# An xLSTM cell in chunks: scores and carried state by two heads at a time on halves of TensorE's rows, q loaded once, narrow matmuls streamed up to 128 columns wide

## The reference, cut to what matters

```python
B, H, S, D = 4, 8, 768, 40
for t in range(S):
    m_new = maximum(f_gate[:, :, t] + m, i_gate[:, :, t])
    f_stab = exp(f_gate[:, :, t] + m - m_new)
    i_stab = exp(i_gate[:, :, t] - m_new)
    m = m_new
    C = f_stab * C + i_stab * outer(v[:, :, t], k[:, :, t])   # 40 x 40 per head
    n = f_stab * n + i_stab * k[:, :, t]
    h = C @ q[:, :, t]
    y[:, :, t] = sigmoid(o_gate[:, :, t]) * h / maximum(abs(n @ q[:, :, t]), 1.0)
x = y as (B * S, H * D)         # 3072 x 320
logits = x @ w_gate             # then routing, experts, second network
```

## Time and profile before

| | |
|---|---|
| median of 3 runs | 818.24 us (818.19 to 818.46) |
| the profiled execution | 816.46 us |
| its span, first to last instruction | 814.7 us |
| PE / PEld busy over the span | 766.5 us (94%) / 719.1 us (88%) |
| DVE / ACT / POOL busy | 585.3 us (72%) / 323.2 us (40%) / 170.4 us (21%) |
| this stage (24 tiles) | about the first 180 us |

### The profile page before, as it was taken

How to read it: one execution, slowest core, us unless ns; L and a number is a source line. 1 busy time by engine, 2 the same in 40 slices (tenths; PEclk the granted TensorE clock), 3 DMA queues, 4 the chain that set the end, 5 groups by cost and what they waited for, 6 DMA issues and landing times.

```text
span 814.7 us, 17195 instructions
## 1 busy us (share of the span) xinstructions
PE 766.5 (94%) x5535; PEld 719.1 (88%) x5535; DVE 585.3 (72%) x1614; ACT 323.2 (40%) x775; POOL 170.4 (21%) x244
## 2 busy tenths in 40 slices
PE   5999999985389999999999999999999999999995
PEld 4999999973378998999899889989998998999995
DVE  5767677776767876887788678768867876884442
ACT  4656566520223442361345145323613442362331
POOL 8257677510100110021002102100210110021001
PEclk9999999965599999999999999999999999999998
DMA  6887887510500500230041005004100500230000
GB/s 157 221 227 214 234 214 215 139 40 2 171 1 1 162 27 10 77 95 24 0 142 29 24 14 157 24 0 141 29 24 0 161 26 8 80 91 25 2 1 24
DMA packets 73408, 65.79 MB, mean 81 GB/s; under 512 B 35232, under 2 KB 64544, under 8 KB 73376
## 3 DMA queue, kind: packets, MB, share of 16 engines
q1 hardware_dynamic: 63584, 51.94, 23.0%
q0 software_dynamic: 2688, 8.65, 3.4%
q10 hardware_dynamic: 7104, 4.79, 1.9%
HBM read 56.71 MB, written 8.65 MB: 80 GB/s over the span
## 4 chain that ended last, share of the span: by engine, by line
PE 91%; DVE 5%; DMA 1%; issue 1%; POOL 0%; ACT 0%; ACTq 0%; DVEq 0%; POOLq 0%
PE bank L835 20%; PE bank L837 18%; PE bank L836 18%; PE bank L677 6%; PE bank L724 5%; PE bank L853 4%; PE bank L854 4%; PE bank L705 2%; PE bank L712 2%; PE bank L688 2%; PE bank L878 1%; PE bank L879 1%; PE bank L669 1%; PE bank L758 1%; PE bank L733 1%
## 5 line engine op out<-in xcount | busy, mean ns | idle before, releaser
L835 PE MATMUL bank<-wo_hi,h_hi 128*128 128x320 f32 x384 | 120.8, 314 | 0.0
L837 PE MATMUL bank<-wo_hi,h_lo 128*128 128x320 f32 x384 | 118.6, 309 | 0.0
L836 PE MATMUL bank<-wo_lo,h_hi 128*128 128x320 f32 x384 | 118.0, 307 | 0.0
L601 POOL DMA_INDIRECT xe<-x_rows,idx_in x24 | 30.5, 1272 | 403.2 <-DVE idx_in L1434 353.9
L1494 DVE SCALAR_TENSOR_TENSOR g_act<-g_neg,rest_alpha,bank 128x384 f32<-128x384 f32 x128 | 78.6, 614 | 39.2 <-ACT g_neg L1066 37.7
L1066 ACT ACTIVATE g_neg<-bank 128x384 f32<-128x384 f32 x128 | 62.8, 491 | 102.0 <-PE bank L854 102.0
L1070 ACT CAST h_hi<-g_act 128x384 fp32r<-128x384 f32 x128 | 65.7, 513 | 78.8 <-DVE g_act L1494 78.3
L1064 ACT ACTIVATE h_hi<-bank 128x384 fp32r<-128x384 f32 x64 | 31.5, 492 | 163.4 <-PE bank L854 163.4
L835 PE MATMUL bank<-yT_hi,wi_hi 128*128 128x384 f32 x256 | 92.3, 361 | 0.3 <-DVE yT_lo L1520 0.3
L836 PE MATMUL bank<-yT_lo,wi_hi 128*128 128x384 f32 x256 | 86.8, 339 | 0.0
L837 PE MATMUL bank<-yT_hi,wi_lo 128*128 128x384 f32 x256 | 86.7, 339 | 0.0
(11 more groups left out here) (229 smaller groups left out, 1816.1 us busy)
## 6 DMA issues: line engine op xcount, KB each, us to landing
s<-w SPq DMA_DIRECT2D x8, 1280.0 KB, 9.2
s<-w SPq DMA_DIRECT2D x8, 1024.0 KB, 5.5
s<-w SPq DMA_DIRECT2D x16, 256.0 KB, 6.3
k_in<-kT SPq DMA_DIRECT2D x24, 160.0 KB
q_wide<-qT SPq DMA_DIRECT2D x48, 80.0 KB
k_row<-k SPq DMA_DIRECT2D x24, 160.0 KB, 3.4
v_in<-v SPq DMA_DIRECT2D x24, 160.0 KB, 4.0
gate_o<-o SPq DMA_DIRECT2D x24, 160.0 KB, 3.1
```

The lines of the kernel that those rows point to most:

```text
L835: pe.matmul(acc, ah, bh, start=start, stop=False, skip_group_check=True)
L836: pe.matmul(acc, ah, bl, start=False, stop=False, skip_group_check=True)
L837: return pe.matmul(acc, al, bh, start=False, stop=stop, skip_group_check=True)
```

## The change

Rows 0 to 63 of TensorE hold the even head of a pair, rows 64 to 127 the odd one (`half_rows`, `head`). The scores are 8 matmuls on 64 rows each, alternating between the halves, 128 columns into a bank for each half. The carried part is 8 matmuls on 64 rows, alternating, each streaming 123 columns (its own 41 and the next 82, which later matmuls overwrite), one half into CARRY and the other into the UPD bank, behind the state's update. The update is 8 matmuls with 40 columns loaded and 41 streamed, on all rows, whose results land on partitions 0 to 39 or 64 to 103. Because the carried part now writes the bank UPD, the wait for `state_ready` moves ahead of it. q is loaded once, into `q_in`; `q_wide`, `own_half` and their memsets go. The outputs stream 128 columns instead of 41, the logits 96 (12 copies) instead of 8. VectorE reads the carried part in two operations, and writes the state in one of 164 columns on 128 partitions.

```diff
@@ sp
-                sp.dma_start(k_in[0:PD, b, :, :], kT[c, b].rearrange("u d y s -> (u d) y s")).then_inc(qk_in[b], 16)
-                for half in range(2):
-                    sp.dma_start(q_wide[D * half:D * half + D, b, half, :, :], qT[c, b, half]).then_inc(qk_in[b], 16)
...
+                for u in range(2):
+                    sp.dma_start(k_in[ROWS * u:ROWS * u + D, b, :, :], kT[c, b, u]).then_inc(qk_in[b], 16)
+                for u in range(2):
+                    sp.dma_start(q_in[ROWS * u:ROWS * u + D, b, :, :], qT[c, b, u]).then_inc(qk_in[b], 16)
...
                 if not first(T, B):
-                    for half in range(2):
-                        sp.dma_start(q_in[D * half:D * half + D, b, :, :].rearrange("d (a u) s -> d a u s", u=2),
-                                     qT[c, b].rearrange("u d (a n) s -> n d a u s", n=2)[half]).then_inc(q_rows_in[b], 16)
@@ pool, constants
             pool.memset(k_in[:, 1, :, :], 0.0)
-            pool.memset(q_wide[:, 1, :, :, :], 0.0).then_inc(wide_zero, 1)
-            pool.memset(k_row[:, :, DM:], 0.0)
-            pool.memset(v_in[:, :, :, D:D1], 1.0).then_inc(consts, 1)
+            pool.memset(q_in[:, 1, :, :], 0.0).then_inc(wide_zero, 1)
+            pool.memset(v_in[:, :, H:, :], 0.0)
+            pool.memset(state[:, :, :], 0.0)
+            pool.memset(v_in[:, :, 0:H, D:D1], 1.0).then_inc(consts, 1)
...
-            pool.memset(q_in[:, :, :, :], 0.0)
-            pool.memset(state[:, :, :, :], 0.0)
...
@@ pool, weigh_values
-                pool.tensor_tensor(fstate[:, n, :, :], state[0:PD, b, :, :], bc(fade[:, c, b, :], 2 * D1),
+                pool.tensor_tensor(fstate[:, n, :, :], of_batch(b), bc(fade[:, c, b, :], D1),
                                    ALU.mult).then_inc(faded, 1)
@@ pe, front
                 for y in range(HP):
-                    ins = pe.matmul(SCORE[y // 2][:, 2 * P * (y % 2):2 * P * (y % 2) + 2 * P], k_in[:, b, y, :],
-                                    q_wide[:, b, :, y, :], start=True, stop=True)
+                    for u in range(2):
+                        ins = pe.matmul(SCORE[u][:, P * y:P * y + P], k_in[half_rows(u), b, y, :], q_in[half_rows(u), b, y, :],
+                                        start=True, stop=True)
@@ pe, router
-                    ins = pe.matmul(YB[:, H * D1:H * D1 + E], xT_sb[:, t, :], wg_sb[:, t, :],
-                                    start=(t == 0), stop=(t == 2))
+                    ins = pe.matmul(LOGITS.rearrange("p (n e) -> p n e", e=E), xT_sb[:, t, :],
+                                    wg_sb[:, t, :].unsqueeze(1).to_broadcast([P, LOGIT_COPIES, E]), start=(t == 0), stop=(t == 2))
@@ pe, back
+                if not first(T, 1) and (not isinstance(T, int) or T <= NT - B):
+                    pe.wait_ge(state_ready, T)
...
                 for y in range(HP if not first(T, B) else 0):
-                    pe.matmul(pair(CARRY[:, 0:H * D1].rearrange("p (h d) -> p h d", d=D1), y), q_in[:, b, y, :], state[:, b, y, :], start=True, stop=True)
+                    for u in range(2):
+                        pe.matmul(CARRIED[u][:, D1 * y:D1 * y + 3 * D1], q_in[half_rows(u), b, y, :],
+                                  state[half_rows(u), HP * b + y:HP * b + y + 3, :].rearrange("p y d -> p (y d)"), start=True, stop=True)
                 pe.wait_ge(kv_in[b], 32 * (c + 1))
                 if not final(T):
                     pe.wait_ge(vw_ready, T + 1)
-                    if not first(T, 1):
-                        pe.wait_ge(state_ready, T)
                 for y in range(HP if not final(T) else 0):
-                    pe.matmul(UPD[:, 2 * D1 * y:2 * D1 * (y + 1)], k_row[:, b, 2 * D * (y // 2 + 2 * (y % 2)):2 * D * (y // 2 + 2 * (y % 2)) + P],
-                              pair(vw[:, n, :, :], y), start=True, stop=True)
+                    for u in range(2):
+                        pe.matmul(UPDATE[ROWS * u:ROWS * u + D, D1 * y:D1 * y + D1], k_row[:, b, D * (HP * u + y):D * (HP * u + y) + D],
+                                  vw[:, n, head(u, y), :], start=True, stop=True)
...
-                        ins = pe.matmul(YB[:, D1 * h:D1 * h + D1], probs[:, n, half, y, :], v_in[:, b, h, :], start=True, stop=True)
+                        h, at = head(half, y), D1 * (HP * half + y)
+                        ins = pe.matmul(YB[:, at:at + WIDE], probs[:, n, half, y, :],
+                                        v_in[:, b, :, :].rearrange("p h d -> p (h d)")[:, D1 * h:D1 * h + WIDE], start=True, stop=True)
@@ dve, make_x
-                    ch.link(dve.tensor_tensor(carried[:, :, :], grid(CARRY), bc(gT[:, c, hs], D1), ALU.mult))
+                    for u in range(2):
+                        ins = dve.tensor_tensor(of_half(carried[:, :, :], u), CARRIED[u][:, 0:HP * D1].rearrange("p (y d) -> p y d", d=D1),
+                                                of_half(bc(gT[:, c, hs], D1), u), ALU.mult)
+                        ch.mark(ins) if u == 0 else ch.link(ins)
...
-                            ins = dve.scalar_tensor_tensor(out=state[0:PD, b, :, cols], in0=new, scalar=own_half[:, half:half + 1],
-                                                           in1=fstate[:, n, :, cols], op0=ALU.mult, op1=ALU.add)
+                        ins = dve.tensor_tensor(of_batch(b), new, fstate[:, n, :, :], ALU.add)
```

More of the change, by code:

```diff
@@ L48, in build_program @@
     REST = DM - 2 * P
-    PD = 2 * D
+    ROWS = P // 2
     J1, J2 = F1 // P, F2 // P
@@ L191, in build_program @@
         wT = ga("wT", [P, NCH, HB])
-        fade = ga("fade", [PD, NCH, B, HP])
-        state = ga("state", [P, B, HP, 2 * D1])
+        fade = ga("fade", [P, NCH, B, HP])
+        state = ga("state", [P, B * HP + 3, D1])
         q_in = ga("q_in", [P, B, HP, P])
-        q_wide = ga("q_wide", [P, B, 2, HP, P])
         k_in = ga("k_in", [P, B, HP, P])
-        k_row = ga("k_row", [P, B, DM + P - PD])
+        k_row = ga("k_row", [P, B, DM])
         gate_o = ga("gate_o", [P, B, DM])
-        own_half = ga("own_half", [PD, 2])
-        v_in = ga("v_in", [P, B, H, D1])
+        v_in = ga("v_in", [P, B, H + 3, D1])
         vw = ga("vw", [P, 2, H, D1])
@@ L360, in pieces_before, with half_rows, head, of_half @@
             return sum(len(first_pieces(i)) for i in range(n))
+        def half_rows(u):
+            return slice(ROWS * u, ROWS * u + ROWS)
+        def head(u, y):
+            return 2 * y + u
+        def of_half(heads, u):
+            return heads.rearrange("p (y u) d -> p u y d", u=2)[:, u, :, :]
+        def of_batch(b):
+            return state[:, HP * b:HP * b + HP, :]
         def bc(ap, n):
@@ L486, in _ @@
             pool.memset(k_in[:, 1, :, :], 0.0)
-            pool.memset(q_wide[:, 1, :, :, :], 0.0).then_inc(wide_zero, 1)
-            pool.memset(k_row[:, :, DM:], 0.0)
-            pool.memset(v_in[:, :, :, D:D1], 1.0).then_inc(consts, 1)
+            pool.memset(q_in[:, 1, :, :], 0.0).then_inc(wide_zero, 1)
+            pool.memset(v_in[:, :, H:, :], 0.0)
+            pool.memset(state[:, :, :], 0.0)
+            pool.memset(v_in[:, :, 0:H, D:D1], 1.0).then_inc(consts, 1)
             for b in range(2, B):
                 pool.memset(k_in[:, b, :, :], 0.0)
-                pool.memset(q_wide[:, b, :, :, :], 0.0).then_inc(wide_zero, 1)
-            pool.memset(q_in[:, :, :, :], 0.0)
-            pool.memset(state[:, :, :, :], 0.0)
[L495 to L502, removed]
+                pool.memset(q_in[:, b, :, :], 0.0).then_inc(wide_zero, 1)
+            ch.link(pool.memset(half_ones[:, :, :], 0.0))
+            pool.memset(half_ones[:, 0, half_rows(0)], 1.0)
+            pool.memset(half_ones[:, 1, half_rows(1)], 1.0).then_inc(consts, 1)
             ch.link(pool.memset(ones_bf[:, :], 1.0))
@@ L667, in front @@
                     for y in range(HP):
-                        h = H * b + HP * half + y
+                        h = H * b + head(half, y)
                         ins = pe.matmul(LOGD[half][:, P * y:P * y + P], sel3[:, h:h + 1].to_broadcast([P, P]),
@@ L1106, in _ @@
             dve.memset(k_in[:, 0, :, :], 0.0)
-            dve.memset(q_wide[:, 0, :, :, :], 0.0).then_inc(wide_zero0, 1)
+            dve.memset(q_in[:, 0, :, :], 0.0).then_inc(wide_zero0, 1)
+            ones_done.mark(dve.memset(UPDATE, 0.0))
             ones_done.mark(dve.memset(peak3[3 * HB:P, :], 0.0))
@@ L1251, in read_logits @@
                 dve.wait_ge(logit_done, T + 1)
-                dve.tensor_copy(logits[:, T, :], YB[:, H * D1:H * D1 + E]).then_inc(logit_read, 1)
+                dve.tensor_copy(logits[:, T, :], LOGITS[:, 0:E]).then_inc(logit_read, 1)
             def make_x(c, b):
@@ L1256, in make_x @@
                 n = b % 2
-                ch = Chain(dve, dve_step, STEP_LINKS * T - (T if first(T, B) else B))
+                ch = Chain(dve, dve_step, STEP_LINKS * T - 2 * (T if first(T, B) else B))
                 hs = slice(H * b, H * b + H)
```

(20 more changed lines are left out.)

41 lines of the change are left out of this document (20 added, 21 removed).

## The result

The median of four runs of the changed kernel is 797.54 us (796.16 to 799.48), beside 818.35 us for the kernel before on the same chip: a ratio of 0.9742, 95% interval 0.9717 to 0.9768. The profiled execution took 797.02 us, where the prediction's sum gave 797.4.

The account below looks back on a forecast made before the run. TensorE was taken to set the loop's pace. Start -6.0, T = 4 to 19 -12.0 (15 rounds of 6.05 us) and end -1.1 took 816.46 us to 797.4, or 799 as median of runs; range 790 to 832.

Parts of the forecast that it names:

- Two halves at once: Scores and carried part on TensorE: halves overlap at 56 ns a matmul, -0.89 us for scores, +0.05 for carried part.
- rival 1: Halves don't overlap; scores and carried matmuls pay 112 ns each, round 7.74 us, total 832 us; chance 0.24.
- Three switches at 0.12 us: Changes between full and half height in TensorE's round: three, together +0.36 us, range 0.2 to 0.45.
- Update 0.58: State's update on TensorE: 16 instructions loading 40 columns take 0.58 us instead of 0.89, -0.31 a round.
- Widening 0: Wider outputs, logits and carried part stay under the load's time: 0 a round, with 0.1 us kept in the range.
- TensorE's round 5.96: Sum of TensorE's terms for one round in the loop: 5.96 us, from 6.75.
- The moved wait just fits: Carried part now waits for the state: ready at about 112.24 us, TensorE there at 112.28.
- Rival 3: VectorE, ScalarE and GpSimd bound the round above 6.05 us; at 6.5 us a round, 806 us; chance 0.10.
- Start -2.6 and -3.4 of clock: Until T = 4: fewer memsets and shorter first scores give -2.6 us, full clock -3.4; together -6.0.
- q once 0: Loading q once saves 160 KB and two issues a tile, off the path: 0.
- Rival 2: Half an overlap, 84 ns each: 6.75 + 0.05 in the loop, only start and clock gains remain, 814 us; chance 0.12.
- Rival 4: TensorE's clock falls more often with 64 rows working; each 3.4 us at half costs 1.7, eleven eat the gain; chance 0.04.

Follow-up runs that it names:

- same_half_in_a_row: The changed kernel with scores and carried part issuing all matmuls of one row half before the other, instead of alternating: 811.64 us, ratio 0.9916.
- logits_narrow: The changed kernel with the router's logits alone narrow again, 8 columns instead of 96: 798.95 us, ratio 0.9782 to the kernel before.
- update_columns_in_a_row: The changed kernel with the state's update going through one column half before the other, instead of alternating: 800.06 us, ratio 0.9765.
- before_wide: The kernel before with outputs of 128 columns and logits of 96, nothing else: 814.76 us, ratio 0.9956.
- after_narrow: The changed kernel with outputs of 41 columns, logits of 8 and carried part of 41, halves kept: 861.38 us, four runs from 834.99 to 878.92.

## Why the prediction was right, step by step

- **Two halves at once**: right, at the low end that I took. Pairs 112 ns apart are 56 ns for each of the 32 matmuls, against the 81 ns from which rival 1 decides. same_half_in_a_row shows the overlap as cause for the scores and the carried part together. The Trainium skill, "TensorEngine Tiling (Array Packing)", Key Properties, says that different tiles work in parallel; the trace agrees (the two of a pair start 6 to 7 ns apart).
- **Three switches at 0.12 us**: too small. Decays to scores costs 0.10 ahead of the first pair and 0.10 behind it, carried to update 0.13, and update to router 0.07 (logits_narrow: 0.69 us of router where it was 0.62), with 0.04 us more inside the update: 0.44, at the upper end of 0.2 to 0.45. These shares are my reading of single starts; no run changes a switch alone.
- **Update 0.58**: too large. The instructions of the two column halves pair up too, which I had not considered: 0.43 us with the switch behind it, against 0.58 + 0.12. update_columns_in_a_row, without the pairs, has 0.62.
- **Widening 0**: too small by 0.13 us a round (5.81 to 5.94). The carried part costs 0.07 of it (1.09 us against 1.02). The outputs and the logits cost 0.06 together and not apart: with the logits alone narrow their group is 0.05 shorter (0.69), the outputs behind it are 0.06 longer (1.87 against 1.81), and the round stays. I had kept 0.1 in the range.
- **TensorE's round 5.96**: measured 5.94. That the sum fits so well is luck: the update with its switch came out 0.27 us below its terms, and scores, carried part, router and outputs together 0.30 above theirs.
- **The moved wait just fits**: right. 1.86 us from the transposes to the carried part (predicted 1.82), the state ready 1.41 us behind the carried product (1.5). It fails to fit only in the fourth round, by 0.34 us.
- **6.05 us a round**: measured 90.19 / 15 = 6.01. Rival 3, 6.5, did not come; the sign that I gave for it, a wait of TensorE on the state over 0.1 us, shows in every fourth round alone.
- **Start -2.6 and -3.4 of clock**: the sum, -6.3, was right and its parts were not. The first outputs end 2.9 us sooner (19.83 to 16.94), and the next four rounds are 3.4 shorter. GpSimd's first work on a tile starts 1.6 us sooner (15.67 to 14.05), where I had reckoned up to 3.9; no run separates it from the shorter scores. The clock's share is not 3.4: before_wide, which has full clock there, gains 1.9 in the four rounds (28.36 to 26.44 us, `y_done` of T = 0 to 4). At full clock TensorE is no longer busy all the time there, 11.08 of 12.00 us from 35 to 47, so a part of what the clock gives back goes into waits.
- **Clock in the loop -1.7**: right, 1.66 us by the two rounds of 6.97 and 8.19 before.
- **End -1.1**: -0.6. VectorE's constants (L1185, 1.90 us at 141.06) come ahead of the probabilities in the shorter round, and TensorE waits 0.33 us for them.
- **q once 0**: not tested by itself. It is one issue less a tile and not two, since k now takes two where it took one. Rival 2 has a slip as well: 84 ns each make a round of 6.85, by the prediction's own terms, and not 6.80, some 0.8 us more in all.
- **Rival 4, given 0.04**, is the step that I misjudged, though it didn't decide the time. I listed the widening as a gain of 3.4 + 1.7 us and the rival as something apart. In fact the halves without the widening do lose the clock, 64 us of it, and the widening is what holds it off. Without this part of the change the forecast would have been wrong by far, and that the change held both parts while this rival stood at 0.04 is luck. What is shown is which widths matter; why the clock falls more easily with half-height scores than in the kernel before, which has narrow outputs too and had only 10 us of the stage at half clock (3.4 of them in the loop), was not separated and stays open.

## What to carry to other kernels

Two half-height float32 matmuls cost one load here if the halves alternate instruction by instruction. That gains where full height streams zeros for longer than the load takes, as the scores did (256 columns, 224 ns). It gains nothing where two heads already share one full-height load, as in the carried part. Each change of height costs 0.1 to 0.2 us, so keep each to one place in a round. Time what is left for the engine that feeds back the state, since the round shrinks under it. And when a stage is made of narrow streams behind wide loads, run it once with the streams widened: what that costs was a few hundredths of a microsecond per group here, and what it saves can be the clock of the whole stage. In this kernel wide outputs alone would have done.

## What was not expected of the hardware

- TensorE's matmuls started out of program order when they used different halves of the rows: L713 at 101.39 us ahead of L684 at 101.49, 101.60 and 101.72, which the program has first.
- The granted clock fell to 0.5 with TensorE busy 48.00 of 48.00 us (after_narrow, 124 to 172 us). A full busy column doesn't show that the clock is safe.
- Column halves overlap as row halves do: pairs 7 ns apart, 27 ns for each matmul of the update with all that lies around it, 38 ns in a row.
- At a change of height the wait lies on both sides of the first pair: 0.10 us ahead of it and 0.10 behind.
